# The attention front of a three-stage kernel rewritten: tiles of 128 tokens, 64 keys per 32-token chunk, head pairs as the unit of work

## The reference

```python
for c in range(24):
    l, r = max(0, 32 * c - 16), min(768, 32 * c + 40)
    k_full = concatenate([mem_k, k[:, :, l:r]]);  v_full = concatenate([mem_v, v[:, :, l:r]])
    s = softmax(q[:, :, 32 * c:32 * c + 32] @ k_full.T / 8)
    out[:, :, 32 * c:32 * c + 32] = s @ v_full
x = out as [3072 tokens, 512]
# second: soft mixture of experts, 8 experts with 4 slots each
logits = x @ phi                      # [3072, 32]
slot_input = softmax(logits over all tokens).T @ x
slot_out = per expert: relu(slot_input @ w1[e]) @ w2[e]     # w1, w2: 8 x 2 MB each
x = softmax(logits over slots) @ slot_out
# third: h = x @ w_in; u = h * softmax(h); out = layernorm(u) * g_ln @ w_out
```

## Time and profile before

| | |
|---|---|
| median of 3 runs | 452.37 us (450.63 to 455.35) |
| profiled execution, first to last instruction (span) | 449.5 us |
| around the span, median less span | 2.9 us |
| first `score` product starts | 11.61 us |
| last `pv` products end | 198.2 us |
| `w1` products start | 215.60 us |
| last `w2` transfer is in | 261.3 us |
| third stage's loop over tiles | from 274.08 us to the end |
| PE / PEld / DVE / ACT / POOL busy | 91% / 73% / 62% / 61% / 18% of the span |

### The profile page before, as it was taken

One profiled execution on the slowest core, in us unless ns is written; L12 is line 12 of the kernel. 1 busy time (PEld: TensorE's weight loads), 2 busy tenths in 40 slices (PEclk: granted clock), 3 DMA queues, 4 the chain that ended last, 5 costly groups with the idle time before them and its releaser, 6 DMA issues.

```text
span 449.5 us, 9776 instructions
## 1 busy us (share of the span) xinstructions
PE 407.0 (91%) x3060; PEld 328.2 (73%) x3060; DVE 279.3 (62%) x592; ACT 272.0 (61%) x587; POOL 81.8 (18%) x215
## 2 busy tenths in 40 slices
PE   3879899999999999985999774999999999999997
PEld 2779888889888989862334222788888888888885
DVE  6568776878687868755810016657657567567551
ACT  4579887889787978651113054555655655655642
POOL 1000210022002110000000029433233233233230
PEclk9999999999999999996799958799999999999999
DMA  6786776667566667595699960011010010110111
GB/s 153 171 207 162 172 194 167 167 162 181 143 162 154 170 163 240 181 408 226 231 387 410 412 240 1 1 47 42 29 47 33 37 47 25 45 47 23 47 47 47
DMA packets 104357, 65.45 MB, mean 146 GB/s; under 512 B 87160, under 2 KB 87416, under 8 KB 104336
## 3 DMA queue, kind: packets, MB, share of 16 engines
q1 hardware_dynamic: 104336, 65.18, 47.6%
HBM read 58.88 MB, written 6.29 MB: 145 GB/s over the span
## 4 chain that ended last, share of the span: by engine, by line
PE 71%; SPq 10%; DVE 7%; issue 4%; DMA 4%; ACT 3%; DVEq 0%; ACTq 0%
PE psum L1078 30%; PE psum L929 8%; PE psum L952 6%; PE psum L1005 5%; PE psum L1092 4%; SPq L344 4%; DMA slot<-in_moe_w_dram 3%; PE psum L845 3%; PE psum L939 3%; PE psum L1065 2%; PE psum L899 2%; PE psum L869 2%; PE psum L875 1%; PE psum L1036 1%; PE psum L882 1%
## 5 line engine op out<-in xcount | busy, mean ns | idle before, releaser
L1078 PE MATMUL psum<-Wh,utH 128*128 128x512 f32 x192 | 77.6, 404 | 0.8 <-DVE utL L807 0.8
L1078 PE MATMUL psum<-Wh,utL 128*128 128x512 f32 x192 | 75.6, 394 | 0.0
L1078 PE MATMUL psum<-Wl,utH 128*128 128x512 f32 x192 | 75.5, 393 | 0.0
L929 PE MATMUL psum<-kG,qT 128*96 128x128 f32 x512 | 71.2, 283 | 3.6 <-ACT kG L505 3.5
L807 DVE TENSOR_TENSOR utL<-psum,utH 128x512 fp32r<-128x512 f32 x48 | 33.1, 691 | 56.0 <-ACT utH L619 56.0
L929 PEld LDWEIGHTS psum<-kG,qT 128*96 128x96 f32 x512 | 59.7, 167 | 9.7 <-issue 6.1
L658 DVE TENSOR_REDUCE nmax<-psum 96x4 f32<-96x512 f32 x64 | 43.8, 684 | 22.9 <-PE psum L929 20.9
L952 PE MATMUL psum<-vw,PT 128*96 128x65 f32 x512 | 53.0, 246 | 0.4 <-ACT PT L542 0.4
L952 PEld LDWEIGHTS psum<-vw,PT 128*96 128x96 f32 x512 | 48.5, 165 | 2.6 <-issue 2.4
L612 ACT ACTIVATE e_sb<-psum,negmax 128x1024 f32<-128x1024 f32 x24 | 26.8, 1117 | 37.4 <-DVE negmax L816 37.4
L665 DVE TENSOR_TENSOR Z<-psum,nmax 96x512 f32<-96x512 f32 x64 | 43.9, 687 | 2.5
(11 more groups left out here) (135 smaller groups left out, 625.4 us busy)
## 6 DMA issues: line engine op xcount, KB each, us to landing
slot<-in_moe_w_dram SPq DMA_DIRECT2D x7, 2048.0 KB, 11.6
ring<-in_moe_w_dram SPq DMA_DIRECT2D x16, 512.0 KB, 3.4
ring<-in_moe_w_dram SPq DMA_DIRECT2D x4, 2048.0 KB, 11.0
qk<-in_q_dram SPq DMA_DIRECT2D x32, 192.0 KB, 3.5
qk<-in_k_dram SPq DMA_DIRECT2D x32, 192.0 KB, 3.7
out_dram<-o_sb SPq DMA_DIRECT2D x24, 256.0 KB, 2.0
vw<-in_v_dram SPq DMA_DIRECT2D x32, 168.0 KB
w_in_sb<-in_moe_w_in_dram SPq DMA_DIRECT2D x1, 2048.0 KB, 10.8
```

Of the source, the lines that this page charges most:

```text
L929: last = pe.matmul(psum[0:QT, n % 2, t * KEYS:(t + 1) * KEYS], qT[:, pair % 2, hh, tt * QT:(tt + 1) * QT], kG[:, pair % 2, hh, tt, :], sta ...
L1078: last = pe.matmul(psum[:, 6 + p, :], a[:, p, c, :], w[:, c, :], start=(c == 0 and a is utH and w is Wh), stop=(c == FC2 - 1 and w is Wl))
```

## The change

The attention part is rewritten and fully written out, with no hardware loop. The unit of work is a head pair: 16 iterations and 5 more to finish. Tiles have 128 tokens (4 chunks). There are no masks: each chunk has its own 64 keys (`kW`) and values (`vW`), with the overlapping windows stored once per chunk. Where a window reaches over an end of the sequence, memory keys stand in and the values and their ones are zero. A product of one chunk has 64 rows, 32 columns of stationary operand and 64 (or 65) moving columns; the two heads lie on the two halves of the rows and write to different banks, the four chunks of a tile write to four quarters of the PSUM partitions. Memory keys and values are put in by POOL. `x` has two buffers in place of the copy `xb`. DVE copies the transposed `x` out of PSUM. ACT copies queries in one instruction and keys in two per pair.

```diff
-CPT = 3
-QT = CPT * CHUNK
-WIN = QT + LEFT + RIGHT
+CPT = P // CHUNK
+WIN = LEFT + CHUNK + RIGHT
...
+            def score(g):
+                pe.wait_ge(q_out, g + 1)
+                pe.wait_ge(kmem_step, 3 * (g + 1))
+                wait(pe, shifted, g)
+                wait(pe, xT_out, g - 2)
+                for t in range(T):
+                    for j in range(CPT):
+                        c = CPT * t + j
+                        for hh in range(2):
+                            rows = slice(hh * D, (hh + 1) * D)
+                            last = pe.matmul(psum[j * CHUNK:(j + 1) * CHUNK, hh, t * KEYS:(t + 1) * KEYS],
+                                             qT[rows, g % 2, c * CHUNK:(c + 1) * CHUNK], kW[rows, g % 2, c, :],
+                                             start=True, stop=True, skip_group_check=True)
+                last.then_inc(scored, 1)
...
+            def mix(g):                 # waits p_out, v_in, vmem_put, x_done; then as score, with PT and vW
...
+            for it in range(ITER):      # PE's order; ITER = 21, G = 16
+                if it < G:
+                    score(it)
+                if 0 <= it - 1 < G:
+                    mix(it - 1)
+                if it + 1 < G:
+                    turn_k(it + 1)      # 8 transposes
+                if 0 <= it - 2 < G:
+                    turn_x(it - 2)      # 6 transposes of 128 x 128; wait x_done, shifted of iteration it
...                                     # it % 4 == 2, from 6: lt.  it % 4 == 3, from 7: colmax
+                if it < G:
+                    turn_p(it)          # 6 transposes; wait exped, p_out
+                if it + 2 < G:
+                    turn_q(it + 2)      # 8 transposes
...                                     # it % 4 == 2: l.  == 3: colall.  == 0, from 8: dsum, slot
+            def wait_bank(pe, job):     # the job before in this bank's order must be copied out
...
+            for it in range(ITER):      # ACT's order
+                if it + 1 < G:
+                    evac_k(it + 1)      # 2 x 672 elements per partition
+                if it < G:
+                    act.wait_ge(shifted, it + 1)
+                    act.activation(Z[:, it % 2], Z[:, it % 2], ACT.Exp).then_inc(exped, 1)
...                                     # copies of lt, exponential of ed
+                if it < G:
+                    act.wait_ge(p_turned, it + 1)
+                    wait(act, pv_done, it - 1)
+                    act.activation(PT[:, it % 2]..., psum[:, 2:4, :]..., ACT.Copy).then_inc(p_out, 1)
+                if it + 2 < G:
+                    evac_q(it + 2)      # 768 elements, both banks at once
...                                     # copies of l, dsum, slot
+            for it in range(ITER):      # DVE's order
+                if it < G:
+                    max_and_shift(it)   # 768 elements each
+                if 0 <= it - 1 < G:
+                    normalise(it - 1)   # 12, 12 and 768 elements
+                if 0 <= it - 2 < G:
+                    evac_x(it - 2)      # 768 elements
...
+            def place_v(g):             # POOL: per head a copy of 8 partitions x 24 x 64 elements
+            def place_k(g):             # POOL: copies of 192, 16 and 8 elements; wait k_out, vmem_put
+            for it in range(G):
+                if it + 1 < G:
+                    place_k(it + 1)
+                    place_v(it + 1)
...
+            for it in range(G):         # SP; before it q0 k0 mem_k q1 mem_v v0 k1 q2 fold phi
+                if it + 3 < G:
+                    load_q(it + 3)      # waits q_turned of it + 1; 2 transfers of 96 x 8 pieces
+                if it + 2 < G:
+                    load_k(it + 2)      # waits k_turned of it; the same
+                if it + 1 < G:
+                    load_v(it + 1)      # waits pv_done of it - 1; per head 48 x 23 + 32 + 8 x 23 pieces
+                load_piece(it)          # 512 KB of w1
...
-            sp.wait_ge(side_done, job_count(B - 1, ("slot",)))
+            sp.wait_ge(q_turned, G)
+            sp.wait_ge(k_turned, 2 * G)
             load_weight(sp, RS)
-            sp.wait_ge(scored, UB * B - 3)
+            sp.wait_ge(scored, G)
             load_weight(sp, RS + 1)
-            sp.wait_ge(scored, UB * B)
+            sp.wait_ge(pv_done, G)
+            sp.wait_ge(slot_mm, B - 1)
             load_weight(sp, RS + 2)
-            sp.wait_ge(pv_done, UB * B)
             load_weight(sp, RS + 3)
-            sp.wait_ge(side_done, job_count(B, ("slot",)))
+            sp.wait_ge(slot_mm, B)
             load_weight(sp, RS + 4)
```

More of the change, by code:

```diff
@@ L184, in program @@
         stored = [sem(f"stored{i}") for i in range(2)]
[L186 to L205, removed]
-            for n in range(-4, UB - 4):
-                step(B, n)
@@ new lines, in turn, with turn_q, turn_k @@
+                    last = pe.transpose(psum[:, 6 + h, 2 + j * PQ:2 + (j + 1) * PQ],
+                                        qk[:, g % 2, i, h * JH + j, :], ident[0:PQ, 0:PQ])
+                return last
+            def turn_q(g):
+                pe.wait_ge(q_in[g % 2], 32 * (g // 2 + 1))
+                for h in range(2):
+                    wait_bank(pe, ("q", g, h))
+                    last = turn(0, g, h)
+                last.then_inc(q_turned, 1)
+            def turn_k(g):
+                pe.wait_ge(k_in[g % 2], 32 * (g // 2 + 1))
+                for h in range(2):
+                    wait_bank(pe, ("k", g, h))
+                    turn(1, g, h).then_inc(k_turned, 1)
@@ new lines, in turn_x @@
+            def turn_x(g):
+                b, n = g // HP, g % HP
+                pe.wait_ge(x_done, g + 1)
+                wait(pe, shifted, min(g + 3, G))
+                for t in range(T):
+                    last = pe.transpose(psum[:, t // TH, t % TH * P:(t % TH + 1) * P],
+                                        xs[b % 2][:, t, n * P:(n + 1) * P], ident[:])
+                last.then_inc(x_turned, 1)
+            turn_q(0)
+            turn_k(0)
+            pe.wait_ge(mk_in, 16 * B)
@@ L897, in side @@
                     for t in range(T):
                         j = t % 4
-                        last = pe.matmul(psum[j * NS:(j + 1) * NS, bank, :], ed[:, t, :], xs[:, t, :], start=(t < 4),
-                                         stop=(t >= T - 4), skip_group_check=True)
-                else:
-                    wait(pe, esp_ready, b)
-                    for j in range(4):
-                        last = pe.matmul(psum[j * NS:(j + 1) * NS, bank, 0:1], esp[:], ones[0:QT, 0:1], start=True,
-                                         stop=True, skip_group_check=True)
@@ L985, in _ @@
-            over_units(pe, unit)
-            pe.wait_ge(side_out, count_through(B, UB - 5) - 1)
+                        last = pe.matmul(psum[j * NS:(j + 1) * NS, 6, :], ed[:, t, :], xs[b % 2][:, t, :],
+                                         start=(t < 4), stop=(t >= T - 4), skip_group_check=True)
+                    last.then_inc(slot_mm, 1)
             pe.wait_ge(acc_step, B)
```

774 lines of the change are left out of this document (337 added, 437 removed).

## The result

The changed kernel takes **476.04 us** (median of 4 runs, 474.44 to 477.12) against 452.71 in the same job: ratio 1.0509, 95% interval 1.0459 to 1.0559. It is slower; forecast was 406, range 393 to 444. The profiled execution has a span of 473.7 us.

The account below looks back on a forecast made before the run. PE was taken as the old bound, transfers as the new iterations' floor. Eight iterations at 7.9 us, eight with extra work, start and last `mix` gave 150.8 against 198.15; gain 46.9, span 402.6, median 406 us, range 393 to 444.

Parts of the forecast that it names:

- The products: `score` and `mix` on PE: 96 instructions of 64 columns each, nearly four at once, 1.35 us each per pair.
- the rival with 28 ns apart: Products on PE: only two overlap, `score` and `mix` 2.7 us each, an iteration 9.7, 443 us; chance 0.15.
- The prices of the elementwise groups: DVE 0.95 us for 768 elements; ACT from PSUM 0.81 for 768, 0.73 for 672; POOL 1.55 for 1536.
- The rival with POOL as the bound: POOL's broadcast copies cost what L439 does, `place_v` takes 9.4 us, an iteration 10.3: 437 us; chance 0.06.
- 7.6 us; by the busy share, 0.72 x 11.66 x 1.12, 9.4. I take 7.9: Transfers per pair, 1.99 MB: two estimates of their time; an iteration takes no less than 7.9 us.
- SP issues some 6 us per pair and has two pairs' lead, so the bound is bandwidth: Transfers in the iterations: SP's issuing doesn't bound them, bandwidth does, at 7.9 us per iteration.
- Can PE start them 14 ns apart?: Products on PE: 1.35 us needs starts 14 ns apart; L904's 8 instructions, 9 apart, were taken as yes.
- The clock: Rival in the iterations: half clock gives 11.4 us each, 473 us; for a third, 430; chances 0.10 part, 0.08 most.
- the tail: From the last `mix` to the first `w1` product: 17.45 us becomes 17.85; its last `slot` 0.85 shorter.
- Waits for ACT's copy of queries: Iterations with extra work: `l`, `colall`, `dsum` wait for bank 6; extra work and waits add 2.4, 1.5, 3.1 us.
- The wait for the exponential: Each iteration: ACT's exponential queues behind the key copies until 2.9 us; PE waits 1.7 us for it.
- The part behind 215.60: From the first `w1` product to the end: left at 233.9 us, moving with that product's start.

Follow-up runs that it names:

- a_half: The changed kernel with half as many product instructions, each covering two tiles' columns (the second tile's result is not attention's); 456.59 us, ratio 1.007.
- a_v56_kfirst: a_v56 with SP issuing a pair's keys ahead of the next one's queries; 452.23 us, ratio 0.998 to the kernel before.
- d_kfirst: a_v56_kfirst with values block by block beside zeros, so `mix` is 48 products of 128 rows and 130 columns for 96; 439.64 us, ratio 0.965.
- d_all: d_kfirst with the new order: `turn_k` ahead of `mix` on PE, the exponential ahead of the key copies on ACT; 437.28 us, ratio 0.965.
- a_v56_half: The changed kernel with the edits of a_v56 and a_half together; 430.22 us, ratio 0.947 to the kernel before.
- a_v2_half: a_v2 with half as many product instructions too (the result is not attention's); 405.27 us, ratio 0.898 to the kernel before.
- a_v56: The changed kernel with value transfers per head of 56 partitions x 22 pieces + 40 + 48, for 48 x 23 + 32 + 8 x 23; 453.25 us, ratio 1.003.
- a_v2: a_v56 with values loaded for the first two pairs only and used for all (the result is not attention's); 436.57 us, ratio 0.964.

## Why the prediction was wrong

**The products: right.** "96 instructions each of `score` and `mix` in about 1.5 us": the timeline above has 96 in 1.17 us at a granted clock of 1.00, 12 ns apart; a `mix` at 0.50 takes 1.62 (at 173.41 us), and the first `score` 1.60 at 1.00. L904's 9 ns were the right evidence; the rival with 28 ns apart didn't happen. The Trainium skill (TensorEngine Tiling (Array Packing), Instruction Overhead) gives about 60 cycles to each matmul, an estimated 25 ns; the trace, with 12 ns, doesn't agree.

**The prices of the elementwise groups: right.** The costliest groups after have DVE's maximum at 958 ns (forecast 950) and the key copies at 729 (730), and POOL's value copies at 1459 (1550):

```profile
L581 DVE TENSOR_REDUCE nmax<-psum 128x12 f32<-128x768 f32 x16 | 15.3, 958 | 90.4 <-PE psum L796 90.4
...
L372 POOL COPY vW<-memV 8x1536 f32<-8x1536 f32 x32 | 46.7, 1459 | 11.1 <-issue 8.2
```

The rival with POOL as the bound is out.

**First failed step: the transfers, "7.6 us; by the busy share, 0.72 x 11.66 x 1.12, 9.4. I take 7.9".** The term is mis-sized. The runs show some 12 us per pair with these shapes (a_half, where PE waits for keys: 12.0 by the rate, 12.2 by the timeline) and 10.4 to 11.0 with the other ones. One end of the bound was bytes at the rate of the start, the other the share scaled by the number of pieces, both of transfers to other partitions. Worked out from the rows, a full share moved 178 / 0.72 = 247 GB/s before, 165 / 1.14 = 145 after, 192 / 1.07 = 179 in a_v56_half. The rate per busy time belongs to the shapes in the queue, and the change brought new ones. "SP issues some 6 us per pair and has two pairs' lead, so the bound is bandwidth" missed that SP is held while it issues to a full queue: 6.14 us for keys alone.

**Second failed step: "Can PE start them 14 ns apart?", answered by "so yes, at least in a short burst".** The sum then takes the burst as the whole. Nothing in it asks where 440 instructions per 7.9 us come from, when the trace before had 208 per 11.66, and L904 had eight in a row. The stops are 42 us in `score` and `mix` of the kernel after. When `mix` has half the instructions and the rest stands, they fall from 32.8 to 15.9 us and the time from 452.23 to 439.64 (a_v56_kfirst to d_kfirst), and in the new order from 17.8 to 1.9 us (to d_all). The name for the wait that the prediction lacked is "issue" in the middle of a run of products.

**The clock: partly as the rival had it.** It fell in the iterations, to which the prediction gave 18 in 100. Its price can be read in the tail, where the stretch 216 to 240 us has 0.72: `slot` products take 3.61 us where earlier, in a stretch at 1.00, they took 1.88 (one of the 12 is missing there):

```profile
182.06 1.88 PE L902 MATMUL psum<-x,ed 128*32 128x512 f32 x11
...
233.71 3.61 PE L902 MATMUL psum<-x,ed 128*32 128x512 f32 x12
```

There are two of them in the tail, both 3.61 us. The first is 1.7 us over the one at 1.00; of the last the forecast had 3.51 - 0.85 = 2.66, so it adds 0.95. That makes an estimated 2.7 of the tail's +5.2 us. Inside the iterations the clock goes with the waiting: from 20 to 140 us PE is busy 81 of 120 us at 0.73 in the kernel after, 89 at 0.85 in d_all, 93 at 0.93 in a_v2_half, where no more than transfers and instructions were taken away. That it only follows the waits is argued and not shown: no kernel here kept the clock up with the waits left in. By the prediction's own prices a low clock for a third of the part is worth 24 us (430 for 406), so the share of the 64.9 us that it adds may be large, and is open.

**Waits for ACT's copy of queries: there, and smaller.** `l`, `colall` and `dsum` wait for it 2.3, 2.0 and 2.0 us in all over the part, two times each, about 1 us a time. The wait for the exponential is there as well: `turn_p` stands 6.9 us for it in ten iterations, where the forecast had 1.7 us in each.

**The part behind 215.60: right.** 233.4 us for 233.9. The fixed cost at the start was 1.6 us short, and the tail 5.2.

With both failed terms relieved, a_v2_half takes 405.27 us for the 406 of the sum. That agreement is luck. Its first `score` starts 1.3 us later than forecast, its tail is 3.2 and what follows 4.4 us longer, and the part from first `score` to last `mix` takes 127.4 us for 137.4. Part of this is that it has hardly any value transfers: the sum counts eight iterations at the transfers' 7.9 us, and with 7.0 in their place it would give 130.2 for the part.

**What stays open:** why the value pieces are slower than those of before even in the shapes of a_v56 (179 to 189 GB/s per full share for 247), how far ahead PE's instructions are fetched, and the clock's own share of the loss.

## What to carry to other kernels

When a change multiplies the instructions of an engine, count them per microsecond in the densest stretch and compare with a stretch of the old trace that ran as dense for as long; a burst of eight proves nothing for 384. When it changes the shapes of transfers, price them by the partitions and pieces that they have, not by the bytes of others, and expect the queue's issuing engine to be held as well. Larger products with zeros in them can be the cheaper ones: the kernel with 48 of 128 rows and 130 columns was 3.3% faster than that with 96 of 64 rows and 65 columns.

## What the runs showed of the hardware

- Quarters of the columns and halves of the rows run together. In a_v2_half's timeline the group behind 48 score products of 128 columns starts 0.75 us after them, 15.6 ns for each, where 0.88 ns per column make 113 ns for one alone: 7.2 at once.

```profile
101.90 0.94 PE L797 MATMUL psum<-kW,qT 64*32 64x128 f32 x48
102.65 0.94 PE L822 MATMUL psum<-vW,PT 64*32 64x130 f32 x48
```

- With 64 columns the same kind are 12 ns apart (96 in 1.17 us), where 56 ns of columns for each, 7.2 at once, would make 7.8. So there the columns alone aren't the limit; what is, no run here shows.
- 48 products of 128 rows and 130 columns on column quarters take 1.54 us in d_kfirst's timeline, 0.4 more than 96 half-row ones, and have fewer stops:

```profile
109.82 1.54 PE L827 MATMUL psum<-vW,PT 128*32 128x130 f32 x48
```

- The longest stop of PE for its own instructions was 6.5 us (137.81 to 144.29 us), at a DMA share of 1.13; its instruction packet ended at 142.83. Such packets took 1.35 us on average from 15 to 200 us in the kernel after, and 0.97 in a_v2, where the DMA engines had less to do.
